# A fused attention and FFT-MLP kernel on one core: the attention result turned back by matmuls with two stacked identities

## What is computed

```python
mask = q_bucket[:, :, :, None] == k_bucket[:, :, None, :]
scores = scale * np.matmul(q, k.transpose(0, 1, 3, 2))
scores = np.where(mask, scores, -1000000000.0)
scores = scores - np.max(scores, axis=-1, keepdims=True)
attn = np.exp(scores)
attn = attn / (np.sum(attn, axis=-1, keepdims=True) + 1e-09)
return np.matmul(attn, v).astype(np.float32)
```

## Time and profile before

| what | value |
|---|---|
| median of 3 runs | 718.14 us (718.07 to 718.44) |
| the profiled execution | 718.99 us |
| its span, first to last instruction | 717.2 us |
| outside the span | 1.8 us |
| PE busy | 707.4 us (99%) |
| PEld busy | 606.0 us (84%) |
| DVE busy | 405.7 us (57%) |
| ACT busy | 342.7 us (48%) |
| POOL busy | 329.2 us (46%) |
| mean granted clock of PE | 0.995 of full speed |

### The profile page before, as it was taken

How to read it: one execution, slowest core, us unless ns; L and a number is a source line. 1 busy time by engine, 2 the same in 40 slices (tenths; PEclk the granted TensorE clock), 3 DMA queues, 4 the chain that set the end, 5 groups by cost and what they waited for, 6 DMA issues and landing times.

```text
span 717.2 us, 10761 instructions
## 1 busy us (share of the span) xinstructions
PE 707.4 (99%) x3746; PEld 606.0 (84%) x3746; DVE 405.7 (57%) x828; ACT 342.7 (48%) x694; POOL 329.2 (46%) x295
## 2 busy tenths in 40 slices
PE   7999999999999999999999999999999999999998
PEld 5899999999999897888888888888888888888876
DVE  5998998999999568432221121212424467744443
ACT  4999999999999665233111111111232433222111
POOL 5688888889979779553000000110053655211100
PEclk8999999999999999999999999999999999999999
DMA  6354555445432123220000001010012110000002
GB/s 183 95 137 109 138 135 144 107 122 142 115 90 79 31 59 117 73 90 30 0 1 1 0 1 45 31 50 0 1 46 87 45 67 15 4 27 16 16 30 88
DMA packets 39508, 45.97 MB, mean 64 GB/s; under 512 B 15546, under 2 KB 26936, under 8 KB 39456
## 3 DMA queue, kind: packets, MB, share of 16 engines
q1 hardware_dynamic: 36016, 41.16, 20.3%
q0 software_dynamic: 3296, 4.09, 2.4%
q10 hardware_dynamic: 144, 0.05, 0.0%
HBM read 29.23 MB, written 3.15 MB: 45 GB/s over the span
## 4 chain that ended last, share of the span: by engine, by line
PE 90%; DVE 6%; issue 1%; POOL 1%; ACT 1%; DMA 0%; DVEq 0%; POOLq 0%; ACTq 0%
PE PS L1035 21%; PE PS L1037 21%; PE PS L1036 21%; PE PS L1128 7%; PE PS L1173 4%; PE PS L1172 4%; PE PS L1191 4%; PE PS L1192 4%; DVE negmax L1422 1%; DVE ETL L1431 1%; PE PS L1283 1%; PE PS L1139 1%; PE PS L1208 1%; DMA const<-in_projb_dram 0%; DVE X L1399 0%
## 5 line engine op out<-in xcount | busy, mean ns | idle before, releaser
L1580 DVE SCALAR_TENSOR_TENSOR HL<-PS,HH 128x512 fp32r<-128x512 f32 x48 | 33.2, 691 | 154.3 <-ACT HH L1021 154.3
L1021 ACT ACTIVATE HH<-PS 128x512 fp32r<-128x512 f32 x48 | 28.7, 598 | 183.4 <-PE PS L1037 183.4
L903 ACT ACTIVATE E<-PS,bias,factor 128x768 f32<-128x768 f32 x96 | 95.5, 994 | 13.9 <-DVE factor L1425 7.7
L1422 DVE TENSOR_REDUCE negmax<-PS 128x1 f32<-128x768 f32 x96 | 91.0, 948 | 13.1 <-PE PS L1173 13.0
L1431 DVE TENSOR_TENSOR ETL<-PS,ETH 128x384 fp32r<-128x384 f32 x192 | 97.2, 547 | 1.3 <-ACT ETH L896 1.2
L896 ACT ACTIVATE ETH<-PS 128x384 fp32r<-128x384 f32 x192 | 83.4, 488 | 2.1 <-PE PS L1128 0.5
L1128 PE MATMUL PS<-ident,E 128*128 128x128 f32 x576 | 79.8, 274 | 0.1
L1035 PE MATMUL PS<-UTH,W 128*128 128x512 f32 x192 | 75.7, 394 | 0.0
L1035 PE MATMUL PS<-W2H,HH 128*128 128x512 f32 x192 | 74.8, 390 | 0.2 <-DVE HL L1580 0.2
L1037 PE MATMUL PS<-UTH,W 128*128 128x512 f32 x192 | 74.8, 390 | 0.0
L1037 PE MATMUL PS<-W2H,HL 128*128 128x512 f32 x192 | 74.7, 389 | 0.0
(11 more groups left out here) (205 smaller groups left out, 1553.8 us busy)
## 6 DMA issues: line engine op xcount, KB each, us to landing
RAW<-in_moe_w_ch_dram SPq DMA_DIRECT2D x32, 256.0 KB, 2.7
QK<-in_qk_dram SPq DMA_DIRECT2D x16, 384.0 KB, 4.3
VR<-in_v_dram SPq DMA_DIRECT2D x16, 192.0 KB, 2.7
out_dram<-fin SPq DMA_DIRECT2D x12, 256.0 KB, 2.0
QM<-TOPH SPq DMA_DIRECT2D x15, 192.0 KB, 2.8
KM<-TOPL SPq DMA_DIRECT2D x15, 192.0 KB, 3.1
TOPL<-QM SPq DMA_DIRECT2D x15, 192.0 KB, 2.7
TOPH<-TOPH SPq DMA_DIRECT2D x15, 192.0 KB, 3.0
```

Of the source, the lines that this page charges most:

```text
L903: nc.scalar.activation(E[:, tile % NE, :], s_bank(tile)[:, 0:S], ACT.Exp, bias=bias[:, t:t + 1], scale=factor[:, t:t + 1], accum_out=esum[ ...
L1422: nc.vector.tensor_reduce(negmax[:, t:t + 1], s_bank(tile)[:, 0:S], AX_X, ALU.max, negate=True).then_inc(s_max, 1)
```

## The change

The three transposes of a back unit become three ordinary float32 matmuls. The stationary operand is the same block of OS, 128 x 128. The moving operand was `ident` with 128 columns; it is now `fold_ident`, 128 x 64: two 64 x 64 identities, one upon the other. Each product so turns the block and adds its upper and lower 64 rows, which are the two value parts. The result is 64 columns wide, ACT's copy is 192 columns instead of 384, and POOL's addition with its wait is gone; `finish` is one multiplication. `fold_ident` is made once by POOL, from the two halves of `ident`, after `split_v(0)`, and PE waits for it once, ahead of the first back unit. ACT's copy now waits for the multiplication (`s_x`) of two units ago, where it waited for the addition (`s_sum`).

```diff
-    OL2 = put("OL2", [P, 2, HALF, P], F32, tail - 4 * 2 * DM)
-    OS2 = put("OS2", [P, HALF, D])
+    OL2 = put("OL2", [P, 2, HALF, D], F32, tail - 4 * 2 * DM)
+    fold_ident = put("fold_ident", [P, D])
...
                 pool.wait_ge(emptied["back"], half + 1)
-                if half:
-                    pool.wait_ge(s_x, half)
-                nc.gpsimd.tensor_tensor(OS2[:], OL2[:, i, :, 0:D], OL2[:, i, :, D:P], ALU.add).then_inc(s_sum, 1)
-                pool.wait_ge(s_sum, half + 1)
                 pool.wait_ge(s_inv, 2 * (h + 1))
-                nc.gpsimd.tensor_tensor(X[:, row:row + HALF, (h % H) * D:(h % H + 1) * D], OS2[:],
+                nc.gpsimd.tensor_tensor(X[:, row:row + HALF, (h % H) * D:(h % H + 1) * D], OL2[:, i],
...
             split_v(0)
+            pool.wait_ge(s_ident, 16)
+            nc.gpsimd.tensor_tensor(fold_ident[:], ident[:, 0:D], ident[:, D:P], ALU.add).then_inc(s_fi, 1)
...
                         if h:
-                            act.wait_ge(s_sum, nth[u] - 2)
-                        nc.scalar.activation(OL2[:, i], blocks(ring(unit_no[u])[:, 0:HC]), ACT.Copy).then_inc(emptied["back"], 1)
+                            act.wait_ge(s_x, nth[u] - 2)
+                        nc.scalar.activation(OL2[:, i], ring(unit_no[u])[:, 0:HALF * D].rearrange("p (a b) -> p a b", b=D), ACT.Copy).then_inc(emptied["back"], 1)
...
                     pe.wait_ge(emptied["pv"], 2 * h + i + 1)
+                    if h == 0 and i == 0:
+                        pe.wait_ge(s_fi, 1)
                     for j in range(HALF):
-                        last = nc.tensor.transpose(bank[:, j * P:(j + 1) * P], OS[:, i, j * P:(j + 1) * P], ident[:])
+                        last = nc.tensor.matmul(bank[:, j * D:(j + 1) * D], OS[:, i, j * P:(j + 1) * P], fold_ident[:], start=True, stop=True)
```

More of the change, by code:

```diff
@@ L343, in program @@
                    "back": sem("s_ol")}
-        s_sum = sem("s_sum")
+        s_fi = sem("s_fi")
         s_x = sem("s_x")
```

## The result

The changed kernel takes 725.21 us (median of 4 runs, 723.73 to 726.37), the kernel before 718.11 us (718.02 to 718.44). The ratio is 1.0097, with a 95% interval of 1.0080 to 1.0114: **7.1 us slower**, where +8.6 (726.7 us) was forecast. The profiled execution took 726.37 us with a span of 724.3 us, 7.1 us more than the span before.

The account below looks back on a forecast made before the run. PE was taken to bound attention: +9.6 us for 29 back units, +0.2 for three ahead of a value product, -1.2 where attention ends, +8.6 on 718.14, so 726.7 us; range 722.5 to 733.0, about 0.8 within.

Parts of the forecast that it names:

- PE bounds attention: Through most of attention, time added on PE is added to the end; savings of POOL and ACT there buy nothing.
- A float32 product is two passes with two full weight loads, 0.11 us each: Back units on PE: 128 weight columns set each pass, so a product costs 0.22 us and a unit 0.66 us.
- +0.33 us a unit, 29 times: Back units in attention without a gap behind them: 0.33 us more on PE each, 9.6 us together.
- The three units ahead of a value product: Units (13,0), (13,1), (14,0): PE gaps behind them swallow 0.8 of 0.99 us, so they cost 0.2 us.
- The end of attention, -1.2 us: Where attention ends: a shorter chain over POOL closes PE's gaps, -1.2 us, bounds 0 and 1.5.
- the weights hide: Rival, back units: a pass costs its 64 columns, 0.055 us; 716.9 us. Chance 0.06, plus 0.03 for 718 to 722.
- one after the other: Rival, back units: load and matmul in sequence, 0.165 us a pass, +0.66 a unit; 737.3 us. Chance 0.09.
- ACT is the bound: Rival, attention: ACT, not PE, is the bound, so its copy savings half hide PE's added time; 722 us. Chance 0.03.
- The end gives nothing: Rival, end of attention: ACT or DVE is late anyway; 727.9 us. Chance 0.74 together with the forecast.

Follow-up runs that it names:

- one-pass kernel: The changed kernel with OS and fold_ident as fp32r, the attention result rounded to fp32r: 715.68 us, 0.9982 of the kernel before; measured again, 0.9966.
- the first experiment: The changed kernel with only 64 of the 128 columns of OS as stationary data in each back-unit product: 725.01 us, 1.0120 of the kernel before.

## Why the prediction was right

- **PE bounds attention**: right. Less work for POOL alone gives 1.5 us, more for PE alone gives all of the loss.
- **A float32 product is two passes with two full weight loads, 0.11 us each**: right, 192 loads of 191 ns, 0.113 us apart, and with 128, 96 and 72 stationary columns the passes go with the weights. Before the run this rested on one row in which weights and columns were equally long.
- **+0.33 us a unit, 29 times**: right in size; the steady distance grew by 0.35. That 25 half heads gave +8.1 against +8.3 is partly luck: 25 x 0.35 is 8.75, and the kernel before had two gaps of 0.3 us that went under the longer units. "No slack" was read from one unit's distances. The list of all 32 starts would have shown them.
- **The three units ahead of a value product**: +0.2 forecast; units 26 to 29 together took +0.3, which is unit 26's own cost, so these three cost nothing.
- **The end of attention, -1.2 us**: the mechanism was right, the term undersized. With three longer units (+1.0) this piece was 0.6 us shorter, so gaps of 1.6 us were filled. That is the idle time of the weight loads in the earlier trace rows, 1.5 us, the upper bound of the term; PE's own rows (0.7) showed less than half of it. The one-pass kernel, with cheap units and the short chain, has this piece at 29.30 us, 1.5 less than before. Seen by the experiments it is not one term: of the chain over POOL alone 1.4 us can be had with cheap units, 0.5 with dear ones.
- **Not foreseen**: -0.5 us behind L1208, and -0.3 at the start. Neither can be put down to the change, since both stretches vary by as much without it; that they brought the total nearer to 7 than to 8 is luck of these executions. They make up half of the difference between +8.6 and +7.1; the larger gain at the end is 0.4 of the rest, and the three units ahead of a product are 0.2.
- **The rivals**: "the weights hide" and "one after the other" both fell by the 0.113 us. "ACT is the bound" fell by attention, which grew by 8.1 us with ACT's work down from 57.69 to 53.55 us in 60. "The end gives nothing" fell by the 1.6 us. The Trainium skill (TensorE: Matmul & The Clock Gate, Part 3, The mechanism) has the rule that a load overlaps matmuls only in other row groups, from which the prediction took 737.3 us; as a general rule it does not hold here, since a load of 0.11 us and a pass of 0.055 in sequence would be 0.165 us. The same section names an exception, a background weight buffer into which a load can go ahead; the 0.113 us agree with that.

## To carry to other kernels

A transpose in float32 is one pass with a cheap weight load, a float32 product of the same block is two passes with a full load each: where the product only reorders or adds a few rows, halving its moving columns buys nothing, because the 128 stationary columns set the pace. Ask of each short matmul what is longer, its weights or its columns. And take work off an engine only after looking who waits for it: 19 us less on POOL were worth 1.5 us, and the 0.33 us put on PE counted in 26 of 32 units; of the other six, three had gaps behind them and three stood where PE waited for a chain.

## What the runs showed that I had not expected

**A stationary block of 64 columns is no bargain.** See the first experiment: the passes halved to 0.056 us, and a gap at each edge of the unit took it back; 72 columns had no gap ahead of the unit and a seam of 0.05 us in all.

**DVE and POOL can hold each other up.** DVE adds DS to X in blocks of 128 x 514 (L1399; in the kernels without POOL's addition L1395) while the first products of the MLP run. Durations (ns min/median/max, first and last start) in the kernel before, the kernel after, the kernel without POOL's addition, and the second measurement of that kernel:

```profile
L1399 DVE TENSOR_TENSOR X<-X,DS x3: 1387/1704/2916, 276.6 to 286.4; 128x514 f32<-128x514 f32 x3
```

```profile
L1399 DVE TENSOR_TENSOR X<-X,DS x3: 1179/1682/1704, 284.2 to 293.8; 128x514 f32<-128x514 f32 x3
```

```profile
L1395 DVE TENSOR_TENSOR X<-X,DS x3: 672/1165/6672, 272.6 to 283.1; 128x514 f32<-128x514 f32 x3
```

```profile
L1395 DVE TENSOR_TENSOR X<-X,DS x3: 1173/1636/1715, 272.5 to 282.1; 128x514 f32<-128x514 f32 x3
```

The one of 6.67 us began at 272.64 us and ended at 279.31, after a row of POOL's subtractions had ended at 278.75. The next such addition took 0.67 us, and there it is POOL whose subtraction lasts 2.98 us instead of 1.34. POOL and DVE in the timeline of that execution:

```profile
277.41 1.34 POOL L703 TENSOR_TENSOR W2L<-RAW,W2H 128x512 fp32r<-128x512 f32 x1
280.75 2.98 POOL L703 TENSOR_TENSOR W<-RAW,W 128x512 fp32r<-128x512 f32 x1 [2.00 <-ACT W L872]
```

```profile
272.64 6.67 DVE L1395 TENSOR_TENSOR X<-X,DS 128x514 f32<-128x514 f32 x1
...
281.32 0.67 DVE L1395 TENSOR_TENSOR X<-X,DS 128x514 f32<-128x514 f32 x1
```

Behind the long one PE waited 1.9 us for DVE's HL, and after this wait its granted clock was 0.73 in the stretch 280 to 285 us (1.2 GHz in part of it), with matmuls of 512 columns 0.63 us long instead of 0.39. From the first matmul of the second product to the end that execution took 3.8 us more than the other (442.68 and 438.83 us), from the same program: the expectation that it is an accident of one execution held. In the kernel before, DVE's longest such addition takes 2.92 us, and PE waits there too:

```profile
283.65 0.50 PE L1035 MATMUL PS<-W2H,HH 128*128 128x512 f32 x1 [0.16 <-DVE HL L1580]
```

In the kernel after this wait is not there; that is the 0.5 us behind L1208, for the matmul ahead of it (283.11 us) starts 16.86 us behind L1208 in both traces, and the one after it (283.99 us) 17.74 us before and 17.31 after. The kernel with plain products of 128 columns, which keeps POOL's additions, doesn't have it either. The gaps of 0.3 us in attention look the same. In the timeline of the kernel before, POOL makes mask rows while DVE's scalar step on einv takes 0.53 us instead of 0.16 (the median) and ends at 160.65, as POOL's row ends at 160.62; the loads then wait for DVE:

```profile
157.69 2.93 POOL L608 TENSOR_SCALAR MR<-MB,const 44x768 fp32r<-44x768 f32 x1
...
160.12 0.53 DVE L1450 TENSOR_SCALAR einv<-esum 128x6 f32<-128x6 f32 x1
```

```profile
163.00 0.12 PEld L1035 LDWEIGHTS PS<-TOPH,projH 128*44 128x44 f32 x1 [0.15 <-DVE ETL L1431]
```

Ahead of the second gap this step takes 0.48 us, and the loads wait 0.16 us for ETL. That both engines share something in memory is argued from these rows, not tested. In the stretch of the 6.67 us the DMA engines were busier too (a share of 0.71 from 275 to 280 us, 0.51 in the second measurement), and no run separates the two.

**The clock near the start differs from one execution to the next of one program.** Busy time of PE, granted clock and DMA by stretch, of the changed kernel's first profile and of its second:

```profile
12.00:14.00 2.00, 2.00 (x8) 0.50 0.97 254
14.00:16.00 2.00, 2.00 (x9) 0.50 0.55 171
```

```profile
12.00:14.00 2.00, 1.71 (x11) 1.00 1.00 215
14.00:16.00 2.00, 1.89 (x11) 1.00 0.38 111
```

In the 2 us from 8 to 10 us PE had been busy 0.95 us in the first and 1.04 in the second. At the lower level of 1.2 GHz for some 6 us the first back unit starts at 31.94 us, at the higher one at 29.75, 2.2 us earlier, with the rest of the two traces alike. This is as much as most of the effects under study here, and it is why they were read from distances inside one trace rather than from totals.
